# A gated linear-attention step in front of two dense layers: the state increments as four full-width matmuls, placed one stage earlier

## The reference, cut to what matters

```
for t in range(S):
    state = alpha[:, :, t, :, None] * state + np.einsum('bhd,bhe->bhde', k[:, :, t], v[:, :, t])
    y[:, :, t] = np.einsum('bhd,bhde->bhe', q[:, :, t], state)
x = y as (tokens, 384)
x = (relu(x @ w1_in) ** 2) @ w1_out
h = x @ w2_in;  out = (h / (1 + exp(-h))) @ w2_out
```

## Time and profile before

| | before |
|---|---|
| time, median of 3 runs | 913.71 us (912.73 to 913.8) |
| time of the profiled execution | 913.71 us |
| its span | 912.1 us |
| PE busy / PEld busy | 891.1 us (98%) / 742.6 us (81%) |
| DVE / ACT / POOL busy | 435.6 / 403.6 / 75.8 us |
| granted TensorE clock | full (1.0) in the whole span |

### The profile page before, as it was taken

One profiled execution on the slowest core, in us unless ns is written; L12 is line 12 of the kernel. 1 busy time (PEld: TensorE's weight loads), 2 busy tenths in 40 slices (PEclk: granted clock), 3 DMA queues, 4 the chain that ended last, 5 costly groups with the idle time before them and its releaser, 6 DMA issues.

```text
span 912.1 us, 12930 instructions
## 1 busy us (share of the span) xinstructions
PE 891.1 (98%) x4882; PEld 742.6 (81%) x4882; DVE 435.6 (48%) x658; ACT 403.6 (44%) x754; POOL 75.8 (8%) x107
## 2 busy tenths in 40 slices
PE   6799999999999999999999999999999999999997
PEld 5587878888888888888888888888888888888897
DVE  7788996687778677664343311312212212212310
ACT  4675554445445444544666632333323323233520
POOL 3564300000000000001123000000000000000000
PEclk9999999999999999999999999999999999999999
DMA  9596343224232432301232300200200201100100
GB/s 168 156 258 141 86 115 86 64 64 112 67 79 67 115 74 64 98 18 51 70 123 89 102 1 1 64 7 1 70 1 13 57 1 36 35 1 0 35 10 29
DMA packets 103571, 59.90 MB, mean 66 GB/s; under 512 B 55600, under 2 KB 95152, under 8 KB 103504
## 3 DMA queue, kind: packets, MB, share of 16 engines
q1 hardware_dynamic: 97056, 51.25, 23.3%
q0 software_dynamic: 2048, 6.29, 2.2%
q10 hardware_dynamic: 4400, 1.48, 0.9%
HBM read 45.02 MB, written 9.44 MB: 60 GB/s over the span
## 4 chain that ended last, share of the span: by engine, by line
PE 95%; SPq 3%; DMA 1%; issue 1%; ACT 0%; DVE 0%; DVEq 0%; ACTq 0%
PE h_ps L733 43%; PE z_ps L747 40%; PE job_ps L765 3%; PE job_ps L664 2%; PE job_ps L717 2%; SPq L357 2%; PE job_ps L713 2%; PE job_ps L675 1%; PE z_ps L765 1%; PE job_ps L686 1%; DMA x_raw<-y_sb 1%; SPq L394 0%; SPq L346 0%; DVE qp L1105 0%; ACT x_hi L997 0%
## 5 line engine op out<-in xcount | busy, mean ns | idle before, releaser
L1191 DVE TENSOR_TENSOR g_lo<-g,g_hi 128x512 fp32r<-128x512 f32 x177 | 121.5, 687 | 357.4 <-ACT g_hi L948 243.0
L733 PE MATMUL h_ps<-x_hi,win_hi 128*128 128x512 f32 x576 | 224.8, 390 | 2.6 <-DVE x_lo L1183 1.8
L733 PE MATMUL h_ps<-x_lo,win_hi 128*128 128x512 f32 x576 | 224.1, 389 | 0.0
L733 PE MATMUL h_ps<-x_hi,win_lo 128*128 128x512 f32 x576 | 224.1, 389 | 0.0
L943 ACT ACTIVATE g<-h_ps 128x512 f32<-128x512 f32 x96 | 57.4, 598 | 232.1 <-PE h_ps L733 232.1
L945 ACT ACTIVATE g<-h_ps 128x512 f32<-128x512 f32 x96 | 57.3, 597 | 183.8 <-PE h_ps L733 161.0
L733 PEld LDWEIGHTS h_ps<-x_hi,win_hi 128*128 128x128 f32 x576 | 108.1, 188 | 25.9 <-DVE x_lo L1183 2.3
L733 PEld LDWEIGHTS h_ps<-x_hi,win_lo 128*128 128x128 f32 x576 | 108.1, 188 | 22.5
L733 PEld LDWEIGHTS h_ps<-x_lo,win_hi 128*128 128x128 f32 x576 | 108.1, 188 | 22.3
L747 PE MATMUL z_ps<-g_hi,wout_hi 128*128 128x512 f32 x288 | 116.4, 404 | 0.0
L948 ACT ACTIVATE g_hi<-g 128x512 fp32r<-128x512 f32 x177 | 111.8, 632 | 5.6
(11 more groups left out here) (135 smaller groups left out, 864.3 us busy)
## 6 DMA issues: line engine op xcount, KB each, us to landing
z_scratch<-z_sb SPq DMA_DIRECT2D x18, 256.0 KB, 2.7
x_raw<-z_scratch SPq DMA_DIRECT2D x6, 768.0 KB, 4.5
v_sb<-in_v SPq DMA_DIRECT2D x44, 96.0 KB, 2.5
out_x<-z_sb SPq DMA_DIRECT2D x80, 48.0 KB, 1.7
nat_a<-in_alpha SPq DMA_DIRECT2D x40, 88.0 KB, 2.2
nat_k<-in_k SPq DMA_DIRECT2D x40, 88.0 KB, 2.2
nat_q<-in_q SPq DMA_DIRECT2D x40, 88.0 KB, 2.3
x_raw<-y_sb SPq DMA_DIRECT2D x34, 96.0 KB, 2.3
```

The lines of the kernel that those rows point to most:

```text
L733: last = nc.tensor.matmul(h_ps[f % 2][:], w[:, f, tile(kk)], x[par][:, kk, :], start=(kk == TILES[0] and n == 0), stop=(kk == TILES[-1] an ...
L1191: nc.vector.tensor_tensor(low, g[f % 2][:], high.bitcast(F32), ALU.subtract).then_inc(g_lo_made, 1)
```

## The change

The tensor engine's `i_stage` makes one matmul per batch instead of two: its weights are all 112 columns of `kp_t`, its moving data the 96 columns of both heads' values. The result has four 48 x 48 blocks per batch, of which two (keys and values of the same head) are used; so `i_bank` holds 384 columns instead of 192, `first_sums` and ScalarE's `i_copy` are twice as wide, and the readers pick their blocks out with a stride. I becomes a stage of its own in `stage_step`: for pairs 4 to 8 in the Y step, ahead of Y, for pairs from 9 on one step ahead of Y, right behind S's step. On VectorE `i_stage` stands in I's step and `state_stage` in Y's step, both ahead of `low_g` and of `kq_stage`. The load of v waits for `y_made` alone.

```
@@ stage_step
-        return {"A": 1, "KQ": 3, "S": 4, "Y": 5}[kind] + 3 * (n - PAIRS)
+        return {"A": 1, "KQ": 3, "S": 4, "I": 5, "Y": 5}[kind] + 3 * (n - PAIRS)
     if n == 2 * PAIRS:
-        return {"A": 13, "KQ": 14, "S": 15, "Y": 16}[kind]
-    return {"A": -21, "KQ": -19, "S": -18, "Y": -16}[kind] + 4 * n
+        return {"A": 13, "KQ": 14, "S": 15, "I": 16, "Y": 16}[kind]
+    return {"A": -21, "KQ": -19, "S": -18, "I": -17, "Y": -16}[kind] + 4 * n
@@ beside
-    return sorted(jobs, key=lambda j: ("S", "A", "Y", "KQ").index(j[0]))
+    return sorted((j for j in jobs if j[0] != "I" or has_state(j[1])), key=lambda j: ("S", "A", "I", "Y", "KQ").index(j[0]))
@@ build
-            first_sums = [sb(f"first_sums{i}", [ROWS, BATCH * HD], F32, early) for i in range(2)]
+            first_sums = [sb(f"first_sums{i}", [ROWS, BATCH * 2 * HD], F32, early) for i in range(2)]
@@ load_v (SP)
-
                 wait(sp, y_made, n - 1)
-                wait(sp, i_made, min(n - 1, LASTP - PAIRS + 1))
@@ first_state (GpSimd); sums (VectorE) likewise
-                    added = first_sums[n % 2][r].rearrange("d (b e) -> d b e", b=BATCH)
+                    added = first_sums[n % 2][r].rearrange("d (b e) -> d b e", b=BATCH)[:, :, h * HD:(h + 1) * HD]
@@ i_stage (tensor engine)
-
                 for b in range(BATCH):
-                    for h, cols in ((0, slice(0, 64)), (1, head_rows(1))):
-                        last = nc.tensor.matmul(i_bank(n)[cols, b * HD:(b + 1) * HD], kp_t[:, b, cols],
-                                                v_tile(n)[:, b, h, :], start=True, stop=True, skip_group_check=True)
+                    last = nc.tensor.matmul(i_bank(n)[0:ROWS, b * 2 * HD:(b + 1) * 2 * HD], kp_t[:, b, :],
+                                            v_tile(n)[:, b], start=True, stop=True)
                 last.then_inc(i_made, 1)
@@ y_stage
                 last.then_inc(y_made, 1)
-                if n >= PAIRS and has_state(n):
-                    i_stage(n)
@@ i_copy (ScalarE)
-                nc.scalar.activation(first_sums[n % 2][:], job_ps[0][0:ROWS, 0:BATCH * HD], ACT.Copy).then_inc(i_copied, 1)
+                nc.scalar.activation(first_sums[n % 2][:], job_ps[0][0:ROWS, 0:BATCH * 2 * HD], ACT.Copy).then_inc(i_copied, 1)
@@ VectorE, loop over the steps
                 for kind, n in beside(F):
                     if kind == "S":
                         s_stage(n)
+                    if kind == "I":
+                        i_stage(n)
+                    if kind == "Y" and has_state(n):
+                        state_stage(n)
                     if kind == "KQ":
                         kq_stage(n)
                 low_g(u, f, g_pair(F), u >= UNITS, NF * u)
                 if F == 0:
                     a_reciprocal(PAIRS)
-                for kind, n in beside(F):
-                    if kind == "Y" and has_state(n):
-                        i_stage(n)
-                        state_stage(n)
```

More of the change, by code:

```diff
@@ L59, in stage_step @@
     if n < 2 * PAIRS:
-        return {"A": 1, "KQ": 3, "S": 4, "Y": 5}[kind] + 3 * (n - PAIRS)
+        return {"A": 1, "KQ": 3, "S": 4, "I": 5, "Y": 5}[kind] + 3 * (n - PAIRS)
     if n == 2 * PAIRS:
-        return {"A": 13, "KQ": 14, "S": 15, "Y": 16}[kind]
-    return {"A": -21, "KQ": -19, "S": -18, "Y": -16}[kind] + 4 * n
+        return {"A": 13, "KQ": 14, "S": 15, "I": 16, "Y": 16}[kind]
+    return {"A": -21, "KQ": -19, "S": -18, "I": -17, "Y": -16}[kind] + 4 * n
 BESIDE = {}
 for _n in range(PAIRS, LASTP + 1):
-    for _k in ("S", "A", "Y", "KQ"):
+    for _k in ("S", "A", "I", "Y", "KQ"):
         BESIDE.setdefault(stage_step(_k, _n), []).append((_k, _n))
@@ L719, in y_stage @@
                 last.then_inc(y_made, 1)
-                if n >= PAIRS and has_state(n):
-                    i_stage(n)
             def stage(kind, n):
-                if n < PAIRS or kind in ("S", "Y"):
+                if n < PAIRS or kind in ("S", "I", "Y"):
                     {"A": a_stage, "K": k_stage, "Q": q_stage, "S": s_stage, "T": t_stage, "I": i_stage, "Y": y_stage}[kind](n)
@@ L1152, in sums @@
                 r = head_rows(h)
-                return i_bank(n)[r, 0:BATCH * HD].rearrange("d (b e) -> d b e", b=BATCH)
+                return i_bank(n)[r, 0:BATCH * 2 * HD].rearrange("d (b e) -> d b e", b=BATCH)[:, :, h * HD:(h + 1) * HD]
             def i_stage(n):
```

## The result

| | before | after |
|---|---|---|
| median | 913.08 us (912.71 to 913.8, 5 runs) | 919.61 us (916.95 to 920.26, 5 runs) |
| profiled execution | 913.71 us, span 912.1 | 917.47 us, span 915.9 |
| PE / PEld busy | 891.1 / 742.6 us | 898.3 / 747.9 us |

A forecast was written before the change was run, and what follows sets the result against it. The prediction took the tensor engine, busy 98% of the span and 95% of the chain, as the bound. 913.71 us plus 4.9 for 13 paid calls of I, all else 0, gave 918.6 us, range 916.2 to 920.6.

The forecast's parts named there:

- What I costs after: One full-width I on PE: eight records 99 ns apart, 0.81 us, which is 0.38 us more than before.
- the line through 64 and 128 weight columns: Record pitch of I, from 56 ns at 64 weight columns and 113 at 128: 99 ns at 112.
- the hand-over: On PE, passing from I to the next product, whose weights are wider: some 0.02 us per I.
- How often it is paid: Of I's 20 calls, 13 (pairs 5, 6 and 9 to 19) pay in full: 13 x 0.38 = 4.9 us.
- The holes: PE's waits for VectorE before S of pairs 5 and 9 swallow the added cost of pairs 4, 7 and 8.
- The hole of pair 9: PE's 1.24 us wait before S takes in 0.76 us from pairs 7 and 8, shrinking to about 0.5.
- That of pair 5: PE's 1.11 us wait before S takes in pair 4's 0.38 us, shrinking to about 0.7.
- the 0.7 us either way: VectorE and GpSimd disturbing each other under the moved order could shift pair 5's wait before S; taken as 0.
- VectorE's new order: Inc and state moved ahead of `low_g` and KQ on VectorE: no added wait on PE, margins grow.
- Moving columns as the bound: Rival: I's 96 moving columns set an 82 ns pitch, weights loaded behind; 3.0 us, 916.7 us; chance 0.19.
- a fixed cost by record: Rival: each PE record of I costs 27 ns to issue, so fewer records gain; 911.0 us; chance 0.03.
- new wait: Rival: VectorE's order, above all in steps 14 and 5, delays PE; +2 us, 920.6 us; chance 0.08.

The follow-up runs named there:

- The two cut kernels: Changed kernel with I from pair 4 on given only 48 moving columns, or only 80 of 112 weight columns; one execution each, 917.35 and 917.97 us.
- the shape alone: Kernel before with I as four full-width matmuls and wider sums, left behind Y, VectorE's order as before; 917.63 us against 914.79, ratio 1.0033.
- the order alone: Kernel before with the change's stages and VectorE order, I's matmuls still in two halves of the array; 918.85 us, ratio 1.0043.
- early-only kernel: Kernel before with full-width matmuls for I of pairs 0 to 3 alone and the wide copy on ScalarE; 912.98 us, ratio 0.9989.

## Why the prediction was right

The direction, the mechanism and the size held. That the median came within 1.0 us is in part luck: three of its five executions had a lower clock in the start, which the sum doesn't have (see *The last microsecond*).

*What I costs after*: 0.81 us was forecast, 0.83 measured from pair 9 on. The pitch is 98 ns behind the first distance, 96 on the mean, where the line through 64 and 128 weight columns gave 99; the hand-over is 0.06 where I had 0.02. The two cut kernels show what was only argued: at 112 columns the load sets the pitch, at 80 the moving data.

*How often it is paid*: the term of 13 x 0.38 = 4.9 measures as 4.52 us for the 11 calls from pair 9 on, 0.41 each. For pairs 4 to 8, where I goes straight into line 709, the shape adds 0.34 each; with pairs 5 and 6 that would make 5.2 (0.68 + 4.52). But between S of pairs 4 and 9 only 0.20 arrived, since VectorE's new order gave about half a microsecond back there, as told below: 0.20 + 4.52 = 4.7.

*The holes* took in pairs 4, 7 and 8: between S of pairs 4 and 9, five more expensive calls, 1.7 us of PE work, moved the mark by 0.20. The hole of pair 9 went from 1.24 to 0.58 us as forecast. That of pair 5 went to 0.33, not 0.7: VectorE's run was 0.4 us shorter. The order did that, not the shape: with the shape alone the hole is 0.74 us, the forecast 0.7, and with the order alone 0.36. DVE, kernel after, behind the reciprocals of pair 5:

```profile
62.69 0.68 DVE L1155 TENSOR_TENSOR inc<-job_ps,state 48x192 f32<-48x192 f32 x2
63.47 0.99 DVE L1164 TENSOR_TENSOR state<-inc,decay_end 48x192 f32<-48x192 f32 x2
64.50 0.69 DVE L1185 TENSOR_TENSOR g_lo<-g,g_hi 128x512 fp32r<-128x512 f32 x1
```

State takes 0.99 us where it took 1.44, and `low_g` is not hit in exchange. With the shape alone it takes 1.45, with the order alone 0.99. That is the 0.7 us either way that the prediction left open; it fell on the good side. GpSimd's work beside it changed too: one of its instructions (line 533 of the kernel before, 128x384) took 2.66 us there before and with the shape alone, and 1.0 us in the changed kernel and with the order alone. That the two slow each other down fits, but no run was made to test it.

*VectorE's new order* was put at nothing for PE. It brought no wait, and it gave about half a microsecond between S of pairs 4 and 9: 79.50 us with the old order (the shape alone), 78.94 with the new. From pair 9 on inc fits in front of `low_g`:

```profile
202.07 0.74 DVE L1155 TENSOR_TENSOR inc<-job_ps,state 48x192 f32<-48x192 f32 x2 [1.66 <-PE job_ps L682]
203.11 0.69 DVE L1185 TENSOR_TENSOR g_lo<-g,g_hi 128x512 fp32r<-128x512 f32 x1 [0.30 <-ACT g L945]
```

*The rivals.* Moving columns as the bound are refuted for this shape by the kernel with 48 of them, and a fixed cost by record by the one with 80 weight columns. No new wait appeared. The Trainium skill ("TensorE: Matmul & The Clock Gate", LDWEIGHTS) gives 93 ns for 112 columns; the trace agrees within 5 ns, with 98 behind the first distance. Its gap of a lone matmul (Back-to-back issue gap) does not describe these fp32 records: it makes 43 ns of 96 columns, an estimate, and the run with 80 weights, where the moving data set the pitch, has 83.

*The last microsecond.* The median of the five is 6.5 us above that of before, the marks give 5.1, or 4.7 without the last stretch. A part is the clock in the start. Executions of the changed kernel came in two groups: 15 of 22 with a mean granted clock of 0.999 or more, median 917.43 us, and 7 with less, 919.53; three of the five timed ones were of the second group. The kernel before has the same groups, 913.2 to 913.6 and 915.2 to 916.2 us by batch, the second in 33 of 56 executions of the experiments' batches. The line between the groups is not sharp: the mean holds also a fall of the clock at the very end, where PE has little to do, and the profiled execution of the early-only kernel has 0.998 by that alone (1.00 to 905 us, 0.77 behind). So medians of few executions can be 2 us off either way. Within the first group the changed kernel is 3.8 to 4.3 us slower by batch, 0.5 to 0.9 us less than the 4.7. I cannot account for the difference; it may lie in the start, and the two pairs of runs that change only the start contradict each other (-0.8 us, and +0.3, in that group, the latter from 3 executions of each).

## What to carry to other kernels

Before two small matmuls in different halves of the array are merged into one wide one, read the distance from start to start of both forms: merging halves the number of instructions and here nearly doubled the time (0.43 to 0.83 us), since the halves had loaded and streamed side by side. Where the moving columns are fewer than the weight columns, as here, price an fp32 matmul by its weight columns. Keep work in halves together, and look for gains where the engine that bounds the kernel waits: moving two small VectorE stages, of two instructions each, behind what PE waited for gave 1.8 us for nothing.

## What the runs showed of the hardware that was not expected

fp32 records have two separate bounds for their pitch. By weight columns: 45 ns for 48 and 58 for 64 (48 moving, in halves), 98 for 112 (48 or 96 moving), 113 for 128 (128 moving, in row halves); by moving columns: 42 ns for 48 (the first distance of the kernel with half the moving columns), 83 for 96, 109 for 128. Going from the full array to halves and back costs PE about 0.36 us for one stage (0.79 against 0.43).

The tensor engine's clock can fall once in the start. Four of the 13 profiles show it, among them one of two of the same kernel. In the order-alone kernel, PE stood 1.92 us before 38.06 and then got 1.2 GHz for a few microseconds; before the change it stood 1.85 us at the same place and kept its clock, so what brings the fall is open. The order-alone kernel, busy by stretch (columns as in the earlier trace rows, the granted clock is the number before the last two), and its PE records:

```profile
38.00:42.00 4.00, 3.94 (x13) 2.46 (x15) 3.09 (x7) 1.49 (x4) 2.36 (x3) 0.57 0.80 228
42.00:60.00 18.00, 18.00 (x119) 14.59 (x119) 13.74 (x15) 14.36 (x30) 11.91 (x10) 1.00 1.04 244
```
```profile
38.06 0.50 PE L730 MATMUL h_ps<-x_hi,win_hi 128*128 128x512 f32 x1 [1.92 <-DVE x_lo L1180]
...
39.55 0.63 PE L730 MATMUL h_ps<-x_lo,win_hi 128*128 128x512 f32 x1
39.98 0.63 PE L730 MATMUL h_ps<-x_hi,win_lo 128*128 128x512 f32 x1
...
43.05 0.40 PE L730 MATMUL h_ps<-x_hi,win_lo 128*128 128x512 f32 x1
43.29 0.39 PE L730 MATMUL h_ps<-x_hi,win_hi 128*128 128x512 f32 x1
```

The records are 0.43 us apart there and 0.23 after: 2.4 GHz is back. The eight or so records in between cost some 1.6 us, an estimate; the kernel before stands idle for 0.58 us in the same stretch, and S of pair 4 came 0.73 us later than in the profile of before. Over all profiles S of pair 4 was at 55.6 to 56.1 us in the four with the fall and at 53.5 to 55.0 in the nine without, on the median 2.1 us apart, about the distance between the two groups.
